# Second gate of a two-layer expert network: the transposed rows become the stationary operand, nine short products a tile

## The chip, the cores and the metric

One core of one Trainium2 chip. The metric is the device time of one launch in microseconds, median of three runs. TensorE multiplies (weight loads shown apart from the matmuls), VectorE and ScalarE move and transform tiles, GpSimd gathers and scatters rows, SyncE issues loads.

## The reference, cut to what matters

```python
logits = x @ w_gate                                    # x: 3072 x 384, w_gate: 384 x 8
noise_scale = np.log1p(np.exp(x @ w_noise))            # w_noise: 384 x 8
noisy_logits = logits + noise_scale * noise
top2 = np.argpartition(-noisy_logits, 2, axis=1)[:, :2]
...
for e in range(E):                                     # 8 experts, 1024 hidden columns
    for k in range(2):
        mask = top2[:, k] == e
        h = np.maximum(x[mask] @ w1[e], 0.0)
        out[mask] += top2_w[mask, k, None] * (h @ w2[e])
```

Ahead of it stand a recurrent attention (4 batches, 8 heads, 768 steps, head width 48) and a first expert layer in which each token goes to one expert. The `x` of the excerpt is that layer's output. All arrays are float32. Both gates must choose the same experts as the float32 reference, so the second gate is computed with split operands: each float32 value is written as a rounded float32r part (`hi`) and the rest (`lo`), and hi x hi, hi x lo and lo x hi are added.

## The kernel before, in words

The kernel has four stages in time: attention in 24 chunks of 128 tokens (to about 178 us), the first expert layer (to about 407), the second gate with its choice and tables (to about 487), and the second expert layer (to the end). There is no planner: every engine has its own hand-written program, and semaphores order the engines. A wait is written into the program of the engine that waits, and an engine works its program strictly in order.

The second gate works on G = 24 tiles of 128 rows and 384 columns (CC = 3 blocks of 128). SyncE loads them in 12 transfers of two tiles into `gx`, a ring of NGL = 3 groups of GT = 4 tiles, once the first layer's rows are all written (`s_rows`). For each tile t:

- `gate_turn(t)` (TensorE, L1585) transposes three blocks into one of three PSUM banks (`gxT_ps`, ring of NGT = 3). It waits for the vector engine's copy of tile t - 3 (`s_gcopy`).
- ScalarE copies the bank to `gx_hi` in float32r (L804), and VectorE subtracts to get `gx_lo` (L1282).
- `gate_product(t)` (TensorE, L1597) follows two tiles behind `gate_turn`. The stationary operand is `gate_split`: 16 columns of weights' high part and 16 of their low part (gate and noise weights together make 16). The moving operand is the transposed tile, 128 columns: three products with `gx_hi` against all 32 columns, three with `gx_lo` against the first 16. The result has logits in rows and tokens in columns, 512 tokens to a bank (banks 2 to 4).
- Every four tiles ScalarE copies such a bank to `logits_T` (L798), and `gate_back` (TensorE, L1607) brings it to tokens in rows: each 128 tokens of `logits_T` are stationary, and `both`, two 16 x 16 identities above one another, is moving. This adds the two halves. It is a float32 product, which TensorE runs in two passes. The result lands in bank 6, 16 columns a tile.

VectorE then reads bank 6 once (L1285, multiplied with the first layer's gate value), and a chain of small instructions on VectorE and ScalarE picks the two experts of each token, counts, and makes the tables that the gathers of the second layer need. SyncE issues the second layer's first weight loads when tile 23 has been turned (L468).

Other lines that the argument uses: L1476 to L1561 are TensorE's attention products, all plain float32; L1561 is the first gate (stationary `y_T` 128 x 128, moving 8 columns), L1499 has 128 moving columns, L1524 has stationary blocks of 64 columns and 48 moving ones, L1545 is a bf16 product with 12 moving columns, L1555 and L1570 are transposes. L1660 to L1662 are the three float32r products of the expert layers.

Of the kernel before, what the change touches and what calls it, by code (L numbers as in the profile page):

```python
# [16 lines left out]
F32 = mybir.dt.float32  # L17
F32R = mybir.dt.float32r
BF16 = mybir.dt.bfloat16
# [8 lines left out]
def attention_moe_moe(nc, HP, D, w_T, kv_T, small_T, modality_T, modality_bias, w1_1, w2_1, w1_2, w2_2, out):  # L28
# [25 lines left out]
    GB = GT * NGL  # L54
    NHOT = 3

    GATE_ORDER = [(0, 0)] + [(1, m) for m in range(CC)] + [(0, m) for m in range(1, CC)]
    assert ET <= EC <= (B - EB) * NC and ES + 3 <= SURE[0] and EB * NC == 12
    assert D < HS and C % P == 0 and NC % (2 * NIN) == 0 and G % GB == 0 and GB % NGT == 0
    CX = C + 2  # L60
# [2 lines left out]
    with ctx:  # L63
        def sb(name, shape, dt=F32):
            return ctx.enter_context(nc.sbuf_tensor(name, shape, dt))
# [41 lines left out]
        gx_lo = [sb(f"gx_lo{i}", [P, CC, P], F32R) for i in range(NGT)]  # L107
        sb("gap", [P, 16])
        gate_split = sb("gate_split", [P, CC, 4 * E], F32R)
        both = sb("both", [4 * E, 2 * E])  # L110
        logits_x = sb("logits_x", [P, G, E])
        logits = sb("logits", [P, G, E])
        tmp_e = sb("tmp_e", [P, G, E])
# [23 lines left out]
        low_i = sb("low_i", [P, 2 * G], I32)  # L137
        low = sb("low", [P, 2 * G], BF16)
        high = sb("high", [P, 2 * G], BF16)
        with nc.sbuf_tensor("logits_T", [4 * E, GB * P], F32) as logits_T, \  # L140
                nc.sbuf_tensor("x_hi", [P, CC, R], F32R) as x_hi, nc.sbuf_tensor("x_lo", [P, CC, R], F32R) as x_lo:
            pass
        low_hot = sb("low_hot", [P, 2 * G, P], BF16)
# [130 lines left out]
        s_gw, s_ghi = sem("s_gw"), sem("s_ghi")  # L274
        s_gload = [[sem(f"s_gload{i}{h}") for h in range(2)] for i in range(NGL)]
        s_gT, s_gcopy, s_gmm = sem("s_gT"), sem("s_gcopy"), sem("s_gmm")
        s_glT, s_gback = sem("s_glT"), sem("s_gback")
        s_route = sem("s_route")
        s_ask = [sem(f"s_ask{l}") for l in range(2)]
        s_answer = [sem(f"s_answer{l}") for l in range(2)]  # L280
# [437 lines left out]
        @block.scalar  # L718
        def _(act):
            prime(act, [s_ktok, s_xl, s_carry, s_ytok])  # L720
            prime(act, [s_glT], NGL)
            prime(act, s_xst, 16)
            act.dma_start(small[:, :], small_T).then_inc(s_u, 16)
            act.dma_start(bias_all[:, :, :], modality_bias.partition_broadcast(P)).then_inc(s_small, 16)
# [62 lines left out]
            for l in range(2):  # L787

                if l == 1:
                    for i in range(2):  # L790
                        act.wait_ge(s_xst[i], 16 + 16 * (G // 2))
                    act.wait_ge(s_ask[0], 1)
                    act.activation(tmp_f[:, :, :], tmp_e[:, :, :], ACT.Exp).then_inc(s_answer[0], 1)
                    def logits_copy(q):
                        act.wait_ge(s_gmm, (q + 1) * GT + NGT)
                        act.wait_ge(s_gback, q + 1)
                        n = q % NGL
                        act.activation(logits_T[:, n * GT * P:(n + 1) * GT * P], ps[0:4 * E, 2 + n, :], ACT.Copy)\  # L798
                           .then_inc(s_glT, 1)

                    for t in range(G):
                        act.wait_ge(s_gT, t + 1)
                        act.wait_ge(s_gmm, t + 1)
                        act.activation(gx_hi[t % NGT][:, :, :], gxT_ps[t % NGT], ACT.Copy).then_inc(s_ghi, 1)  # L804
                        if t >= GT and t % GT == NGT - 1:
                            logits_copy(t // GT - 1)
                    logits_copy(G // GT - 1)
                    act.wait_ge(s_ask[1], 1)
                    act.activation(tmp_f[:, :, :], raw2[:, :, E:2 * E], ACT.Exp).then_inc(s_answer[1], 1)
                    act.wait_ge(s_answer[1], 1)  # L810
                    act.activation(scale2[:, :, :], tmp_f[:, :, :], ACT.Ln, bias=1.0).then_inc(s_answer[1], 1)
                    act.wait_ge(s_ask[1], 2)
                    act.activation(exp2[:, :], denom[:, :], ACT.Exp).then_inc(s_answer[1], 1)

                def row_hot(q):
                    part = slice(q * G, (q + 1) * G)
                    act.wait_ge(s_is[l], q + 1)
                    last = act.activation(high_hot[:, part, 0, 0:NTX[l]], high_is[:, part, 0:NTX[l]], ACT.Copy,
                                          scale=row_1[:, 0:1])
                    if l == 1:  # L820
                        for g in range(q * G + G // 2, (q + 1) * G):
                            last = act.activation(high_hot[:, g, 1, 0:NTX[l]], high_is[:, g, 0:NTX[l]], ACT.Copy,
                                                  scale=float(g))
                    last.then_inc(s_hota[l], 1)


                def hidden_high(s, q):
                    act.wait_ge(s_h[l], s * 4 + q + 1)
                    act.activation(hid_hi[:, 2 * q:2 * q + 2, :], h_ps[q], ACT.Relu).then_inc(s_hhi[l], 1)  # L829

                def step_slot(j, u):
                    s = j * 2 + u
                    if not runs_from(l, s):
                        for q in range(4):
                            hidden_high(s, q)
                        if s == 0:
                            row_hot(0)
                        return
                    hidden_high(s, 0)
                    if isinstance(s, int) and s == (ES - 1, 0)[l]:  # L840
                        act.wait_ge(s_table[l], (2, 3)[l])
                    run = lookup(act, slot_run[l], s, E - 1)
                    change, fresh = lookup(act, w1_now[l], s, 1), lookup(act, w2_now[l], s, 1)
                    for q in range(4):
                        if q:
                            hidden_high(s, q)
                        with act.If(change > 0):
                            split_w1(l, run + 1, q)
                    with act.If(fresh > 0):
                        if not isinstance(s, int) or s > 0:  # L850
                            act.wait_ge(s_o[l], s * 2)
                            act.nop(nofuse=True)
                        for a in (1, 0):
                            split_w2(l, run + 1, a)

                if l == 1:
                    row_hot(0)
                    for q in range(4):
                        split_w1(1, 0, q)
                    row_hot(1)  # L860
                    for a in (1, 0):
                        split_w2(1, 0, a)
                slots(act, l, step_slot, 2)
# [3 lines left out]
        def _(dve):  # L867
# [184 lines left out]
            def gate_parts():  # L1052

                dve.wait_ge(s_const, 5)
                dve.wait_ge(s_u, 16)
                link(dve.tensor_copy(gate_split[:, :, 0:2 * E], gate_w[1][:, :, :]))
                link(dve.tensor_tensor(gate_split[:, :, 2 * E:4 * E], gate_w[1][:, :, :], gate_split[:, :, 0:2 * E],
                                       ALU.subtract))
                link(dve.tensor_tensor(both[:, :], ident[0:4 * E, 0:2 * E], ident[0:4 * E, 2 * E:4 * E], ALU.add))
                dve.sem_inc(s_gw, 1)  # L1060

            def pick_best(at, end):
# [210 lines left out]
            for l in range(2):  # L1273
                K, NSl, KG = TOPK[l], NTX[l], TOPK[l] * G

                if l == 1:
# [3 lines left out]
                    for t in range(G):  # L1280
                        dve.wait_ge(s_ghi, t + 1)
                        dve.tensor_tensor(gx_lo[t % NGT][:, :, :], gxT_ps[t % NGT], gx_hi[t % NGT][:, :, :],  # L1282
                                          ALU.subtract).then_inc(s_gcopy, 1)
                    dve.wait_ge(s_gback, NGL + G // GT)
                    link(dve.tensor_tensor(raw2[:, :, :], ps[:, 6, 0:G * 2 * E].rearrange("p (g e) -> p g e", e=2 * E),  # L1285
                                           gate1[:, :].unsqueeze(2).to_broadcast([P, G, 2 * E]), ALU.mult))
                    dve.sem_inc(s_ask[1], 1)
# [172 lines left out]
        def _(pe):  # L1460
            prime(pe, [s_y], 2)
            prime(pe, [s_gmm], NGT)
            prime(pe, [s_gback], NGL)
            pe.wait_ge(s_const, 3)

            def head_on(tile, h):
# [109 lines left out]
            for l in range(2):  # L1576
# [11 lines left out]

                def gate_product(t):

                    q = t // GT
                    if t % GT == 0:
                        pe.wait_ge(s_glT, q + 1)
                    pe.wait_ge(s_gcopy, t + NGT + 1)
                    for n, (lo, m) in enumerate(GATE_ORDER):
                        rows = 2 * E if lo else 4 * E
                        last = pe.matmul(ps[0:rows, 2 + q % NGL, (t % GT) * P:(t % GT + 1) * P],  # L1597
                                         gate_split[:, m, 0:rows], (gx_lo if lo else gx_hi)[t % NGT][:, m, :],
                                         start=(n == 0), stop=(n == 2 * CC - 1))
                    last.then_inc(s_gmm, 1)  # L1600

                def gate_back(q):

                    pe.wait_ge(s_glT, q + NGL + 1)
                    for t in range(q * GT, (q + 1) * GT):
                        at = (t - q * GT + q % NGL * GT) * P
                        last = pe.matmul(ps[:, 6, t * 2 * E:(t + 1) * 2 * E], logits_T[:, at:at + P], both[:, :],  # L1607
                                         start=True, stop=True)
                    last.then_inc(s_gback, 1)

                if l == 1:
                    pe.wait_ge(s_gw, 1)
                    for t in range(G + NGT - 1):
                        if t < G:
                            gate_turn(t)
                        if t >= NGT - 1:
                            gate_product(t - (NGT - 1))
                        if t >= GT + NGT and t % GT == NGT % GT:
                            gate_back((t - NGT) // GT - 1)
                    gate_back(G // GT - 1)  # L1620

                if l == 1:
                    pe.wait_ge(s_chosen[1], 1)
# [172 lines left out]
```

## Time and profile before

| | us |
|---|---|
| median of three runs (lowest, highest) | 985.83 (985.77, 986.16) |
| the profiled execution's own time | 985.47 |
| its span, first to last instruction | 983.7 |
| TensorE matmuls busy | 906.2 (92%) |
| VectorE busy | 540.5 (55%) |
| ScalarE busy | 230.3 (23%) |
| GpSimd busy | 349.9 (36%) |
| mean granted TensorE clock | 0.967 |

The profile is of one execution. PE is TensorE's matmuls, PEld its weight loads, which overlap with matmuls; a matmul's duration contains its latency, so the distance between starts of like instructions says more of the rate than the duration. DVE is VectorE, ACT ScalarE, SP SyncE. The granted clock is 1.00 at 2.4 GHz and 0.50 at 1.2 GHz.

### The profile page before, as it was taken

What the parts mean: (1) busy time and instruction counts of PE and PEld (TensorE: products, weight loads), DVE (VectorE), ACT (ScalarE), POOL (GpSimd) and SP (SyncE); (2) the same over time, 40 slices, a digit from 0 to 9 for tenths busy, and PEclk for the clock granted to TensorE, in tenths of its full rate; (3) what the DMA queues carried; (4) which work ended last, traced back from release to release, by engine and by line L of the source; (5) the groups of instructions that cost most, each with busy time, mean ns of one, the idle gap of its engine ahead of it and who ended that gap; (6) DMA issues with size and microseconds to landing.
All of it is one profiled execution on the core that took longest, in us unless ns stands there. A gap on an engine that the chain in (4) does not pass through costs nothing.

```text
span 983.7 us, 22470 instructions
## 1 busy us (share of the span) xinstructions
PE 906.2 (92%) x7285; PEld 876.3 (89%) x7286; DVE 540.5 (55%) x968; ACT 230.3 (23%) x435; POOL 349.9 (36%) x364
## 2 busy tenths in 40 slices
PE   5999999999999999591499999999999999999995
PEld 5888887999999999591399999999999999999995
DVE  8888999784333343257663544435435454443532
ACT  2232333112011121054221222203213131221210
POOL 7333334324221313101542433423443424334232
PEclk9999999999999999895699999999999999999998
DMA  6676782219111112253253534525334443522233
GB/s 250 193 229 228 257 289 92 65 44 390 50 50 33 56 40 57 69 178 119 50 186 73 122 103 112 110 36 127 96 56 104 115 109 108 116 33 52 47 48 50
DMA packets 54594, 111.69 MB, mean 114 GB/s; under 512 B 8704, under 2 KB 35712, under 8 KB 54528
## 3 DMA queue, kind: packets, MB, share of 16 engines
q1 hardware_dynamic: 34896, 71.27, 21.7%
q0 software_dynamic: 15744, 34.70, 17.3%
q10 hardware_dynamic: 3888, 4.89, 1.4%
q8 instruction: 35, 0.57, 0.3%
q14 instruction: 31, 0.25, 0.1%
HBM read 84.84 MB, written 26.00 MB: 113 GB/s over the span
## 4 chain that ended last, share of the span: by engine, by line
PE 82%; DVE 12%; issue 3%; DMA 1%; DVEq 1%; ACT 1%; POOL 0%; POOLq 0%
PE ps L1660 22%; PE ps L1662 21%; PE ps L1661 21%; PE ps L1570 3%; PE ps L1530 2%; PE ps L1534 2%; PE ps L1476 2%; DVE grow L898 2%; PE ps L1499 2%; PE ps L1561 1%; DVE scores L913 1%; PE ps L1585 1%; PE ps L1597 1%; PE ps L1524 1%; DVE rest L883 1%
## 5 line engine op out<-in xcount | busy, mean ns | idle before, releaser
L1660 PE MATMUL ps<-x_hi,weights 128*128 128x256 f32 x984 | 279.1, 284 | 4.6 <-DVE x_lo L1374 2.6
L1662 PE MATMUL ps<-x_hi,weights 128*128 128x256 f32 x984 | 278.5, 283 | 0.0
L1661 PE MATMUL ps<-x_lo,weights 128*128 128x256 f32 x984 | 278.2, 283 | 0.0
L829 ACT ACTIVATE hid_hi<-ps 128x512 fp32r<-128x512 f32 x164 | 98.0, 598 | 539.7 <-PE ps L1662 533.1
L1379 DVE SCALAR_TENSOR_TENSOR hid_lo<-ps,hid_hi 128x512 fp32r<-128x512 f32 x164 | 112.8, 690 | 194.2 <-ACT hid_hi L829 172.5
L1660 PE MATMUL ps<-weights,hid_hi 128*128 (+1 forms) x616 | 214.2, 348 | 1.2 <-DVE hid_lo L1379 1.2
L1662 PE MATMUL ps<-weights,hid_lo 128*128 (+1 forms) x616 | 207.3, 336 | 0.0
L1661 PE MATMUL ps<-weights,hid_hi 128*128 (+1 forms) x616 | 207.2, 336 | 0.0
L1660 PEld LDWEIGHTS ps<-x_hi,weights 128*128 128x128 f32 x984 | 187.4, 190 | 6.6 <-issue 6.5
L1661 PEld LDWEIGHTS ps<-x_lo,weights 128*128 128x128 f32 x984 | 187.4, 190 | 0.0
L1662 PEld LDWEIGHTS ps<-x_hi,weights 128*128 128x128 f32 x984 | 187.2, 190 | 0.0
L563 POOL COPY src_now<-src_row 128x2 int32 (+1 forms) x44 | 11.3, 257 | 304.3 <-DVE row_mix L1366 174.9
L1660 PEld LDWEIGHTS ps<-weights,hid_hi 128*128 128x128 f32 x616 | 115.7, 188 | 2.2 <-issue 1.6
L1661 PEld LDWEIGHTS ps<-weights,hid_hi 128*128 128x128 f32 x616 | 115.8, 188 | 0.0
L1662 PEld LDWEIGHTS ps<-weights,hid_lo 128*128 128x128 f32 x616 | 115.5, 188 | 0.0
L677 POOL DMA_INDIRECT out_dram<-sy,dst_now x56 | 89.8, 1604 | 47.2 <-DVE sy L1392 29.8
L567 POOL DMA_INDIRECT sx<-moe_rows,src_now x62 | 64.9, 1047 | 35.0 <-POOL src_now L563 24.8
L1372 DVE CAST x_hi<-ps 128x384 fp32r<-128x384 f32 x86 | 47.4, 552 | 27.2 <-PE ps L1570 27.0
L1392 DVE TENSOR_TENSOR sy<-ps,row_mix 128x384 f32<-128x384 f32 x56 | 28.6, 553 | 48.8 <-PE ps L1662 48.7
L1570 PE MATMUL ps<-ident,sx 128*128 128x128 f32 x258 | 43.2, 277 | 11.2 <-DMA sx<-moe_rows,src_now 8.8
L1374 DVE TENSOR_TENSOR x_lo<-ps,x_hi 128x384 fp32r<-128x384 f32 x86 | 48.0, 558 | 3.0
L636 POOL TENSOR_TENSOR weights<-stage,weights 128x1536 f32 (+1 forms) x9 | 31.5, 3500 | 50.1 <-ACT weights L782 50.1
(281 smaller groups left out, 1064.4 us busy)
## 6 DMA issues: line engine op xcount, KB each, us to landing
stage<-in_moe_w_dram SPq DMA_DIRECT2D x18, 1536.0 KB, 8.2
kv_in<-in_kv_T_dram SPq DMA_DIRECT2D x24, 512.0 KB, 5.7
kv_in<-in_kv_T_dram SPq DMA_DIRECT2D x24, 448.0 KB, 3.4
w_in<-in_w_T_dram SPq DMA_DIRECT2D x24, 258.5 KB, 4.2
out_dram<-zeros SPq DMA_DIRECT2D x26, 192.0 KB
x_rows<-y_tok ACTq DMA_DIRECT2D x24, 192.0 KB
stage<-moe_rows SPq DMA_DIRECT2D x12, 384.0 KB, 4.2
stage<-in_moe_w_dram SPq DMA_DIRECT2D x2, 768.0 KB, 7.7
```

Of the source, the lines that this page charges most:

```text
L567: pool.indirect_dma_start(out=sx[u][:, t, 0:width], out_offset=None, in_=rows, in_offset=bass.IndirectOffsetOnAxis(ap=src_now[u][:, t:t + ...
L636: pool.tensor_tensor(weights[:, bass.ds(to + W2_LO, HALF)], w2_raw[:, HALF:WSZ], weights[:, bass.ds(to + W2_HI, HALF)], ALU.subtract).then ...
L677: pool.indirect_dma_start(out=out, out_offset=where, in_=sy[u][:, t, 0:C], in_offset=None, compute_op=ALU.add).then_inc(s_scatter[l][u][t] ...
L829: act.activation(hid_hi[:, 2 * q:2 * q + 2, :], h_ps[q], ACT.Relu).then_inc(s_hhi[l], 1)
L1372: dve.tensor_copy(x_hi[:, :, part], x_T).then_inc(s_xhi[l], 1)
L1374: dve.tensor_tensor(x_lo[:, :, part], x_T, x_hi[:, :, part], ALU.subtract).then_inc(s_sxc[l], 1)
L1379: dve.scalar_tensor_tensor(hid_lo[:, part, :], h_ps[q], 0.0, hid_hi[:, part, :], ALU.max, ALU.subtract).then_inc(s_hlo[l], 1)
L1392: dve.tensor_tensor(sy[u][:, t, 0:C], o_ps[t], row_mix[:, bass.ds(s * TS + t, 1)].to_broadcast([P, C]), ALU.mult).then_inc(s_oc[l], 1)
L1570: last = pe.transpose(x_T[:, c, :], sx[u][:, t, c * P:(c + 1) * P], ident[:, :])
L1660: pe.matmul(out_ps, hi, by_hi, start=first, stop=False)
L1661: pe.matmul(out_ps, hi, by_lo, start=False, stop=False)
L1662: return pe.matmul(out_ps, lo, by_hi, start=False, stop=final)
```

## The change

`gate_product` swaps its operands. The transposed tile (`gx_hi` or `gx_lo`, one block of 128 x 128) is stationary, and 16 columns of `gate_split` move. For each of the three blocks there are three products: hi with the weights' high part, hi with their low part, lo with their high part; nine accumulate in bank 6, tokens in rows. `gate_back`, `logits_copy`, `logits_T`, `both` and the semaphores `s_glT` and `s_gback` go. VectorE's read of bank 6 now waits for the last `gate_product`. The tensor `first_half` only keeps the place in memory that `logits_T` had; the tensors behind `both` move by 64 bytes a partition.

```diff
-    GATE_ORDER = [(0, 0)] + [(1, m) for m in range(CC)] + [(0, m) for m in range(1, CC)]
+    GATE_ORDER = [(x, w, m) for m in range(CC) for x, w in ((0, 0), (0, 1), (1, 0))]
...
-        both = sb("both", [4 * E, 2 * E])
...
-        with nc.sbuf_tensor("logits_T", [4 * E, GB * P], F32) as logits_T, \
+        with nc.sbuf_tensor("first_half", [P, G, P], BF16), \
...
-                    def logits_copy(q):
-                        act.wait_ge(s_gmm, (q + 1) * GT + NGT)
-                        act.wait_ge(s_gback, q + 1)
-                        n = q % NGL
-                        act.activation(logits_T[:, n * GT * P:(n + 1) * GT * P], ps[0:4 * E, 2 + n, :], ACT.Copy)\
-                           .then_inc(s_glT, 1)
...
-                        if t >= GT and t % GT == NGT - 1:
-                            logits_copy(t // GT - 1)
-                    logits_copy(G // GT - 1)
...
-                link(dve.tensor_tensor(both[:, :], ident[0:4 * E, 0:2 * E], ident[0:4 * E, 2 * E:4 * E], ALU.add))
...
-                    dve.wait_ge(s_gback, NGL + G // GT)
+                    dve.wait_ge(s_gmm, NGT + G)
...
-                    q = t // GT
-                    if t % GT == 0:
-                        pe.wait_ge(s_glT, q + 1)
                     pe.wait_ge(s_gcopy, t + NGT + 1)
-                    for n, (lo, m) in enumerate(GATE_ORDER):
-                        rows = 2 * E if lo else 4 * E
-                        last = pe.matmul(ps[0:rows, 2 + q % NGL, (t % GT) * P:(t % GT + 1) * P],
-                                         gate_split[:, m, 0:rows], (gx_lo if lo else gx_hi)[t % NGT][:, m, :],
-                                         start=(n == 0), stop=(n == 2 * CC - 1))
+                    for n, (x, w, m) in enumerate(GATE_ORDER):
+                        last = pe.matmul(ps[:, 6, t * 2 * E:(t + 1) * 2 * E], (gx_hi, gx_lo)[x][t % NGT][:, m, :],
+                                         gate_split[:, m, w * 2 * E:(w + 1) * 2 * E],
+                                         start=(n == 0), stop=(n == 3 * CC - 1))
                     last.then_inc(s_gmm, 1)
...
-                def gate_back(q):
-
-                    pe.wait_ge(s_glT, q + NGL + 1)
-                    for t in range(q * GT, (q + 1) * GT):
-                        at = (t - q * GT + q % NGL * GT) * P
-                        last = pe.matmul(ps[:, 6, t * 2 * E:(t + 1) * 2 * E], logits_T[:, at:at + P], both[:, :],
-                                         start=True, stop=True)
-                    last.then_inc(s_gback, 1)
...
-                        if t >= GT + NGT and t % GT == NGT % GT:
-                            gate_back((t - NGT) // GT - 1)
-                    gate_back(G // GT - 1)
```

## Rows read from the trace of the kernel before

**Rows 1.** The page: TensorE's busy tenths in 40 slices of 24.6 us.

```profile
PE   5999999999999999591499999999999999999995
```

**Rows 2.** The chain that ended last, 417 to 446 us: start, us, what.

```profile
418.10 2.24 PE ps L1585 x9
...
426.14 0.36 PE ps L1597 x6
426.50 0.33 PE ps L1585 x3
...
428.61 1.01 PE ps L1607 x8
...
430.11 0.36 PE ps L1597 x6
...
441.52 0.84 PE ps L1597 x12
...
443.03 1.07 PE ps L1607 x8
...
444.13 0.57 DVE raw L1285
```

**Rows 3.** Instructions in order of time, 424 to 441 us, VectorE and SyncE.

```profile
426.70 1.94 DVE L1282 TENSOR_TENSOR gx_lo<-ps,gx_hi 128x384 fp32r<-128x384 f32 x3 [1.19 <-ACT gx_hi L804]
...
440.18 0.38 SPq L413 DMA_DIRECT2D stage<-in_moe_w_dram  x1
```

**Rows 4.** Weight loads by line and shape: count, busy us, mean ns, idle before.

```profile
L1660 PEld LDWEIGHTS ps<-x_hi,weights 128*128 128x128 f32 x984 | 187.4, 190 | 6.6 <-issue 6.5
...
L1561 PEld LDWEIGHTS ps<-small,y_T 128*128 128x128 f32 x192 | 23.3, 192 | 2.2 <-issue 2.2
...
L1555 PEld LDWEIGHTS ps<-ident,y_T 128*128 128x128 f32 x96 | 10.9, 142 | 2.9 <-DVE y_T L967 2.4
...
L1597 PEld LDWEIGHTS ps<-gx_hi,gate_split 128*32 128x32 f32 x72 | 6.7, 110 | 0.9 <-issue 0.3
...
L1545 PEld LDWEIGHTS ps<-early_hot,low_hot 128*128 128x128 bf16 x12 | 0.4, 96 | 0.0
```

**Rows 5.** TensorE in order of time, attention stage, 60 to 68 and near 160.

```profile
65.62 0.97 PEld L1561 LDWEIGHTS ps<-small,y_T 128*128 128x128 f32 x8
...
66.54 1.14 PE L1499 MATMUL ps<-rk,u_block 128*128 128x128 f32 x8
...
160.15 0.45 PE L1545 MATMUL ps<-early_hot,low_hot 128*128 128x12 bf16 x12
```

**Rows 6.** Stretches in the gate: us, PE busy (count), granted clock, DMA share, GB/s.

```profile
418.10:420.90 2.80, 2.80 (x15) 0.50 1.04 373
420.90:421.20 0.30, 0.30 (x5) 0.71 1.08 405
421.20:424.60 3.40, 3.40 (x45) 1.00 1.01 323
```

**Rows 7.** The same columns for stretches of attention and first experts.

```profile
138.00:140.00 2.00, 1.13 (x11) 1.00 1.08 401
...
162.00:164.00 2.00, 0.92 (x9) 1.00 0.00 0
...
165.10:168.40 3.30, 3.30 (x27) 0.50 0.16 55
...
176.00:178.00 2.00, 1.45 (x12) 1.00 0.45 139
...
178.80:182.10 3.30, 3.30 (x18) 0.50 0.49 136
```

**Rows 8.** Weight loads in order of time, half clock, then full.

```profile
11.71 1.83 PEld L1499 LDWEIGHTS ps<-rk,u_block 128*128 128x128 f32 x8
13.77 0.94 PEld L1524 LDWEIGHTS ps<-kv_in,k_tok 128*64 128x64 f32 x16 [0.23 <-issue]
...
61.00 0.55 PEld L1524 LDWEIGHTS ps<-kv_in,k_tok 128*64 128x64 f32 x16 [0.28 <-issue]
```

More of the change, by code:

```diff
@@ L276, in attention_moe_moe @@
         s_gT, s_gcopy, s_gmm = sem("s_gT"), sem("s_gcopy"), sem("s_gmm")
-        s_glT, s_gback = sem("s_glT"), sem("s_gback")
         s_route = sem("s_route")
@@ L720, in _ @@
             prime(act, [s_ktok, s_xl, s_carry, s_ytok])
-            prime(act, [s_glT], NGL)
             prime(act, s_xst, 16)
@@ L1462, in _ @@
             prime(pe, [s_gmm], NGT)
-            prime(pe, [s_gback], NGL)
             pe.wait_ge(s_const, 3)
```

## The prediction

> **What bounds the kernel now.** I read the page's slices first: TensorE is at 9 tenths nearly throughout, but slices 17 to 20 read 5, 9, 1, 4 [rows 1]. Those slices lie between the two expert layers, where the second gate works. Whatever its length, everything behind it (noise, choice of two experts, tables, first gathers) starts when its logits are in PSUM, and no expert product can run before that. So the change is worth what it does to the interval from the first turned tile (418.10) to the vector engine's read of the logits (444.13), one for one.
>
> The chain of waits through that interval [rows 2] is TensorE's own work and nothing else. The reader is to see a pattern: 0.33 us for three transposes (L1585), 0.36 for the six products of a tile (L1597), and after every fourth tile 1.01 us for eight passes that turn the logits back (L1607), behind which the next transposes start slowly: four tiles take 430.11 - 426.14 = 3.97 us, 4 x 0.69 + 1.2. At the end, 12 products (0.84), a gap to 443.03 in which ScalarE makes its last copy, and eight more passes (1.07). The vector engine's subtraction (L1282) keeps pace; three of them last 1.94, so one starts each (1.94 - 0.56) / 2 = 0.69 us [rows 3]. It is paced by the tiles; its own work is 0.56.
>
> **What is taken away.** Six groups of turning passes at 1.2 us beside the transposes, of which the last is 1.07 alone, and the last copy with its hand-over (441.52 + 0.84 = 442.36 to 443.03, 0.67): 5 x 1.2 + 0.67 + 1.07 = 7.7 us. Also the six products of each tile, 0.36. The five other ScalarE copies lie beside TensorE work and give nothing. The vector instruction that made `both` (32 x 16 elements) stood in the first expert layer, where TensorE is at 9 tenths with its own products [rows 1] and VectorE's small work lies beside them: nothing; without that cover it would be some 0.2 us. No DMA is moved. The weight load that SP issues behind the last transpose (440.18, [rows 3]) stood 3.95 us ahead of the read of the logits; now three tiles' products lie between, at least as long at either clock, so it starts no later against all that follows.
>
> **What is added.** Nine products a tile with 128 x 128 stationary data and 16 moving columns. The trace has no such float32r product, so its spacing is bounded from neighbours. The stationary load is what must be paid each time. Float32r loads of 128 columns last 190 ns in the expert loop and the plain float32 loads of L1561 192; the gate's own loads of 32 columns last 110 [rows 4]. So float32r loads like float32, by columns. L1561 is the near twin, a full stationary tile with 8 moving columns: 8 loads in 0.97, (0.97 - 0.19) / 7 = 0.111 us each [rows 5]. L1607 gives the same (8 in 1.01 to 1.07, a matmul's latency in it, [rows 2]). Upper bound at this clock: the same loads with 128 moving columns, L1499, (1.14 - 0.28) / 7 = 0.124 [rows 5]. Lower bound: the bf16 products of L1545, 12 in 0.45, (0.45 - 0.17) / 11 = 0.026 [rows 5]; their loads last 96 ns, not 190 [rows 4]. I take 0.11, by the twin. A tile is then 3 + 9 = 12 x 0.11 = 1.32 us where it was 0.69. (If a transpose's load, 142 against 192 ns [rows 4], lets it start earlier, 1.26; with 0.124, 1.45.)
>
> The Trainium skill, page "TensorE: Matmul & The Clock Gate", section on LDWEIGHTS, gives the load as columns over 1.2 GHz, 107 ns for 128; with that figure a tile would be about 1.3 us by estimate, and the twin's 0.111 agrees. The same page, on fast weight load, says that loads of 128 weights that are not FP32 go faster; the 190 ns row speaks against counting float32r among them, and by that rule the sum would fall below today's (rival 2).
>
> *Sum at 2.4 GHz.* Turned tiles 0 to 2 unchanged, to 420.34. The clock is half until about 421.1 (0.50 up to 420.9, 0.71 in the next 0.3 us, [rows 6]), so tile 0's nine cost about 1.4 us. Then 21 tiles x 1.32 = 27.7, the last two 18 x 0.11 = 2.0, a matmul's latency 0.2: 420.34 + 31.3 = 451.6, which is 7.5 us later than 444.13.
>
> **The clock.** This is where I had to choose. The granted clock rises near 421.1 after nine transposes and the first 128-column products, and stays 1.00 while TensorE streams 128 columns in every instruction of a tile [rows 6]. In the changed kernel only 3 of 12 instructions of a tile stream 128 columns; 9 stream 16, and the array waits for loads. What does such a stretch do? The trace has none longer than 0.9 us, but two places come near. At 162 to 165, after a pause (0.92 busy of 2.00), the eight short products of L1561 lead, and the clock is at 0.50 from 165.1, though 128-column passes had begun behind them. At 176.0 to 178.8 TensorE runs four transposes, the eight short products, a pause and the first expert products: 0.50 again [rows 7]. Both times the clock came back behind solid 128- and 256-column passes (3.30 busy of 3.30). Against that, the stretch from 138, with a longer pause (1.13 busy of 2.00) and the same short products, but with eight 128-column passes whole behind them, kept 1.00 [rows 7]. I read these as: what lifts and holds the clock is streaming, and a load with 16 columns behind it is poor in that. Each near place has idle time, so this is a reading and no proof; the other reading (busy is enough) is rival 1.
>
> At 1.2 GHz, loads of 128 columns start 0.213 us apart: L1499 near 12 us, 8 loads in 1.83, (1.83 - 0.34) / 7. Those also stream 128 columns; a row where the load alone counts is L1524, whose pairs of 64-column loads come (0.94 - 0.22) / 7 = 0.103 apart at half clock against (0.55 - 0.14) / 7 = 0.059 at full [rows 8], so 128 columns are about 0.206. I take 0.213. Transposes are 0.213 to 0.249 (nine in 2.24, [rows 2]). Tile: 12 x 0.213 = 2.56 us, between 2.45 and 2.66.
>
> *Sum at 1.2 GHz.* In the kernel before, tile 0's six 128-column products and the next transposes came just ahead of the rise; now short ones stand there, so I expect no rise at all in the gate. 420.34 + 9 x 0.213 (1.9) + 21 x 2.56 (53.8) + 18 x 0.213 (3.8) + 0.35 latency = 480.2. That is 36.1 us later. Behind it TensorE pauses in either kernel, and the later stages keep their rows. VectorE (0.56 a tile, [rows 3]) and the ScalarE copy ahead of it lie beside 2.56. Loads of the rows have more time than they need.
>
> The profiled execution took 985.47 us (span 983.7, 1.8 around it), 0.36 under the median 985.83. 985.47 + 36.1 = 1021.6; against the median 1021.9. I forecast **1022 us**, 3.7% slower. Own range: tile 2.45 to 2.66 gives 21 x 0.1 = 2.2 us either way, with the start and the rise another 2: 1018 to 1026.
>
> **Rivals.**
> 1. *The clock rises at 421 and stays.* For: TensorE has practically no idle time in the new gate, and the falls seen all had pauses. Against: the near places above. Time: +7.5 us, 993.3, with tiles of 1.26 to 1.45 giving 992 to 996. The Trainium skill, same page, section on why this matters for your kernels, says that an engine kept continuously busy goes to full speed and pauses take it back; by that rule this rival holds, with 993 us. The rows above do not decide it: no stretch there is both free of pauses and full of short products.
> 2. *Float32r loads of 128 columns go fast.* One mechanism, the other sign. From 420.34 to 444.13 there are 23.8 us; 21 x 3 x 0.11 = 6.9 are transposes, leaving 16.7 for about 216 product slots: below 0.077 us each the change wins. At the bf16 row's 0.026 a tile's TensorE work would be 0.56, and VectorE's pace of at most 0.69 would bind: 420.34 + 0.6 + 21 x 0.69 + 0.6 = 436, 8 us faster, 978; at 0.06 about 3 us faster, 982.5. Against: 190 ns in [rows 4], the same as float32.
> 3. *The clock goes up and down within the gate,* for stretches with transposes bunched. Half and half: about +22, 1008.
>
> **Chances.** Forecast 0.60, rival 1 0.28, rival 3 0.06, rival 2 0.04; 0.02 for spacing that happens to meet today's time. To leave out at most 2 in 10 the range has to reach rival 1: 991.5 to 1026. What a measurement here can tell from no change is about 0.2%, 2 us. Faster 0.04, same 0.02, slower 0.94: every case but rival 2 adds more than 7 us.
>
> **What would show it.** In the profile after: the loads of L1597's successor, 216 of them (9 x 24) with 128 columns, 0.33 us long at half clock or 0.19 at full; the granted clock from 421 to the end of the gate, 0.50 (forecast) or 1.00 (rival 1); the interval from the first transpose to the read of the logits, 62 us, 33.5 us, or under 26 (rival 2); no wait on ScalarE or VectorE inside it. Everything ahead of 418 and behind the read keeps its length within 1 us. The prediction is wrong if the clock holds, if the loads are not 0.11 or 0.21 apart, or if the stage behind the gate changes length because loads of the second layer's weights now come at another time.

## The result, and the profile after

| | before | after |
|---|---|---|
| median, us (lowest, highest; runs) | 986.0 (985.77, 989.17; 4) | 1021.63 (1020.89, 1022.34; 4) |
| ratio, with its 95% interval | | 1.033 (1.031 to 1.036) |
| the profiled execution's own time | 985.47 | 1022.22 |
| its span | 983.7 | 1020.5 |

The changed kernel is 3.3% slower; its 1021.63 us lie 0.4 under the forecast of 1022. I read its profile in the order of the one before. First the page: TensorE's busy line and, under it, the granted clock, in 40 slices.

```profile
PE   6999999999999999598259999999999999999995
...
PEclk9999998999999999655569999999999999999998
```

A slice is now 25.5 us. In [rows 1] slices 17 to 20 read 5, 9, 1, 4; now slices 17 to 21 read 5, 9, 8, 2, 5: TensorE works for some one slice and a half longer between the two expert layers (944.1 us busy against 906.2, both from the page), and the clock line shows fives there. The chain of waits says with what (start, us, what):

```profile
409.79 0.57 DVE sy L1376
...
417.16 4.70 DMA stage<-moe_rows
...
421.90 0.90 PE ps L1570 x3
422.81 1.72 PE ps L1578 x9
424.52 0.75 PE ps L1570 x3
425.28 1.72 PE ps L1578 x9
...
473.99 0.75 PE ps L1570 x3
474.75 5.57 PE ps L1578 x27
480.34 0.57 DVE raw L1271
```

L1570 is `gate_turn`, L1578 the new `gate_product`, L1271 the vector engine's read of the logits. The pattern of [rows 2], 0.33 and 0.36, has become 0.75 and 1.72, one tile each 2.47 us, twenty-one times without a gap and without an entry of ScalarE or VectorE between. The chain puts the border between two groups where one ends; the starts of the instructions give the terms more plainly (TensorE in order of time, a transpose group, the first products behind it, the next transposes):

```profile
441.69 0.90 PE L1570 MATMUL ps<-ident,stage 128*128 128x128 f32 x3
442.24 0.57 PE L1578 MATMUL ps<-gate_split,gx_hi 128*128 128x16 f32 x2
...
444.16 0.90 PE L1570 MATMUL ps<-ident,stage 128*128 128x128 f32 x3
```

From the first of the nine products to the next transposes it is 1.92 us, 0.213 a product, and the three transposes take 0.55. The view of the tile `gate_split` gives the loads and products one by one (duration lowest/median/highest in ns, first and last start, shape):

```profile
L1578 PEld LDWEIGHTS ps<-gate_split,gx_hi x144: 333/333/337, 422.4 to 479.7; 128*128 128x128 f32 x144
...
L1578 PEld LDWEIGHTS ps<-gate_split,gx_lo x72: 333/333/333, 422.8 to 479.9; 128*128 128x128 f32 x72
```

All 216 loads last 333 ns, from the first to the last; none shows the 190 ns that such a load has at 2.4 GHz [rows 4]. The granted clock in two stretches of the gate (us, busy and count of PE, PEld, DVE, ACT, POOL, granted clock, DMA share, GB/s):

```profile
424.60:430.00 5.40, 5.40 (x28) 5.40 (x27) 1.11 (x2) 0.98 (x2) 0.00 (x0) 0.50 0.60 186
440.00:450.00 10.00, 10.00 (x51) 10.00 (x50) 2.23 (x4) 1.96 (x4) 0.00 (x0) 0.50 0.25 79
```

TensorE is busy for every microsecond of them, as is its weight load, and the clock is 1.2 GHz. Busy is meant as the profile counts it: a product here lasts 0.361 us in the trace and the next one starts after 0.213, so the row is full although, as the experiments below show, each product waits for a load.

**The sum against the profile.** Cut at the first `gate_product` (420.34 before, from [rows 2], 422.81 after) and at the read of the logits (444.13 and 480.34): ahead of the cut +2.47 us; between, 57.53 against 23.79, +33.74; behind, 541.88 against 541.34 to the end of the execution, +0.54. Together 36.75, which is 1022.22 - 985.47. The forecast had 0, 59.9 - 23.8 = +36.1, and 0. So the gate was 2.3 us shorter than forecast and the rest 3.0 us longer, under a total that is right to 0.7 us.

The 2.47 us came before the gate. The last instruction of the first layer's sums starts at 409.79; in the trace of before it started at 407.05. TensorE is already 2.7 us later at the first expert product (181.08 against 178.34), so the time was lost in the attention. Three rows of TensorE's windows of after, for stretches of the attention (us, PE busy and count, clock, DMA share, GB/s):

```profile
138.00:140.00 2.00, 1.28 (x12) 1.00 1.10 405
140.50:143.80 3.30, 3.30 (x27) 0.50 0.95 307
...
164.40:170.90 6.50, 6.50 (x42) 0.50 0.09 33
```

and the second stretch in the kernel before:

```profile
140.50:143.80 3.30, 3.30 (x44) 1.00 0.92 304
```

In [rows 7] the stretch from 138 kept its clock in the kernel before; here the clock is lost behind it, and 27 instructions fit where 44 did. The fall near 165 of [rows 7] lasts 6.5 us in place of 3.3. At the first gate's products behind the pause of 162 the kernel after is 1.1 us late (164.20 against 163.08), and 2.7 at the first expert product. The instructions of that stage are the same in both; only the place of some tensors differs, by 64 bytes a partition. The traces of the experiments below, whose code there is that of the kernel after, put the last instruction of the sums at 406.39 to 411.59, and in one of them, six_wide, the clock did not fall between 136 and 186 us (all engines):

```profile
136.00:186.00 50.00, 43.40 (x481) 38.35 (x480) 44.94 (x65) 17.06 (x39) 24.42 (x22) 1.00 0.42 139
```

The repeated runs of the kernel before alone went from 985.2 to 992.5 us. The variation between runs is enough to explain the 2.7 us; nothing here shows a part of the change in it.

### The profile page after: what moved, and what is told of

Read it like the earlier page. It is cut to its first block, busy times and chain, and to the rows that moved or that the text cites. A ratio compares the mean times of both kernels' runs of the same rounds, so it can differ in the third digit from the quotient of the medians.

```text
span 1020.5 us, 22497 instructions
## 1 busy us (share of the span) xinstructions
PE 944.1 (93%) x7309; PEld 915.2 (90%) x7310; DVE 540.3 (53%) x967; ACT 227.8 (22%) x429; POOL 347.9 (34%) x364
## 4 chain that ended last, share of the span: by engine, by line
PE 84%; DVE 9%; issue 2%; DMA 1%; DVEq 1%; ACT 0%; POOL 0%; POOLq 0%; SPq 0%
PE ps L1629 21%; PE ps L1631 21%; PE ps L1630 21%; PE ps L1578 4%; PE ps L1555 3%; PE ps L1515 2%; PE ps L1519 2%; PE ps L1484 2%; PE ps L1461 2%; PE ps L1570 2%; PE ps L1546 2%; PE ps L1509 1%; DVE grow L885 1%; PE ps L1469 1%; PE ps L1540 1%
```

## The experiments

Three theories are tried: **load** (nine stationary loads are the tile's length, at whatever clock is granted), **streaming** (the clock stays at 1.2 GHz because 16 columns behind a load are poor in streaming; my forecast), **busy** (a TensorE without pauses keeps or gets 2.4 GHz; rival 1). All but the one named otherwise start from the kernel after. The kernel before, timed beside them on the same chip, took 988.51 us with lift, lift_hold, wide and bf16_rows, 987.62 with wide256, six_loads, six_wide and back_twice, and 988.47 with bf16_again; it was 986.0 with the kernel after. The ratios are against these, and a difference of two times from different groups is uncertain by some 2 us.

**1. lift.** Fifty bf16 products of 512 columns ahead of the gate, so that it begins at 2.4 GHz.

```diff
                 if l == 1:
+                    for n in range(50):
+                        pe.matmul(ps[:, 2, :].rearrange("p (a b) -> p a b", a=4), ones_b[:, :],
+                                  causal_b[:, :].unsqueeze(1).to_broadcast([P, 4, P]), start=True, stop=True)
                     pe.wait_ge(s_gw, 1)
```

> The changed kernel with 50 bf16 products of 512 moving columns into an unused bank, run while TensorE waits for the gate's first rows, so that the gate begins at the full clock. Theory (nine loads with 16 columns behind each neither lift nor hold the clock): the granted clock is 1.00 at the gate's start and falls to 0.50 inside it, most of the 24 tiles still take 2.4 to 2.5 us; 1017 to 1021 us. Rival (busy is enough to hold it, only the rise was missed): 1.00 through the gate, tiles of 1.25 to 1.32 us, about 991 us.

One run: 1028.11 us. The windows, all engines:

```profile
432.40:435.90 3.50, 3.44 (x32) 3.44 (x32) 1.50 (x4) 1.10 (x3) 0.00 (x0) 1.00 0.19 22
436.10:440.00 3.90, 3.90 (x21) 3.90 (x20) 0.92 (x2) 0.87 (x2) 0.00 (x0) 0.50 0.44 165
440.00:487.00 47.00, 47.00 (x229) 47.00 (x228) 10.03 (x18) 8.44 (x18) 0.00 (x0) 0.50 0.21 62
```

and the chain of waits:

```profile
411.56 6.04 issue
417.60 13.29 PE ps L1585 x50
430.89 0.34 PE ps L1570 x3
431.26 0.50 ACT gx_hi L794
...
431.85 0.57 DVE gx_lo L1268
...
433.63 0.40 PE ps L1570 x3
434.04 0.91 PE ps L1578 x9
...
436.35 0.75 PE ps L1570 x3
437.11 1.72 PE ps L1578 x9
```

The first row is TensorE before the fillers (here L1585), the next the fillers themselves, and then tiles at either clock. At 2.4 GHz a tile is 0.40 + 0.91 = 1.31 us, the 1.32 of the forecast's sum for that clock; at 1.2 GHz it is 2.47 again. By the starts, the tile at 2.4 GHz is 0.30 us of transposes and 1.01 of nine products, 0.112 each:

```profile
433.49 0.54 PE L1570 MATMUL ps<-ident,stage 128*128 128x128 f32 x3
433.79 0.37 PE L1578 MATMUL ps<-gate_split,gx_hi 128*128 128x16 f32 x2
...
434.80 0.55 PE L1570 MATMUL ps<-ident,stage 128*128 128x128 f32 x3
```

The clock fell at about 436 though TensorE had been busy for 3.44 of the 3.50 us ahead, and did not come back in 47 us of unbroken work. The fall alone would leave a doubt, since the fillers and the first products are parted by a pause of half a microsecond in which ScalarE and VectorE make the first operands (431.26 to 432.42 in the chain, with transposes in part of it). The 47 us behind it leave none. That refutes the busy theory: work without pauses was not enough to give the clock back. The time missed its expectation for another reason: the fillers started 6 us after the last expert product and took 13.29 us, so the gate's first product began at 432.46, 9.7 us later than in the kernel after (422.81).

**2. lift_hold.** The same, and one more such 512-column product behind each tile's nine.

```diff
                             gate_product(t - (NGT - 1))
+                            pe.matmul(ps[:, 2, :].rearrange("p (a b) -> p a b", a=4), ones_b[:, :],
+                                      causal_b[:, :].unsqueeze(1).to_broadcast([P, 4, P]), start=True, stop=True)
```

> As lift, and one bf16 product of 512 columns (0.22 us at full clock) behind every tile's nine. Theory: the added streaming holds the clock at 1.00, a tile takes 1.25 to 1.32 plus 0.22 to 0.25, some 1.5 us, and the kernel is faster than the changed one although it does more: 996 to 1000 us. If the short products pull the clock down whatever stands beside them: tiles of 2.9 us, 1031 us. If busy is enough (rival), also about 998, but then lift is at 991.

1031.98 us, ratio 1.044 (1.041 to 1.047). A miss for streaming as I had sized it; the other case of the expectation (the clock falls all the same, tiles of 2.9 us, 1031) came. The windows:

```profile
428.60:432.10 3.50, 3.46 (x31) 3.31 (x31) 1.48 (x3) 0.78 (x3) 0.00 (x0) 1.00 0.16 9
...
436.00:491.00 55.00, 55.00 (x255) 51.30 (x254) 10.04 (x18) 8.84 (x18) 0.00 (x0) 0.50 0.18 56
```

The clock fell at 432.1, no later in the gate than in lift. The long product of a tile did not hold it; it adds 0.47 us a tile less what the transposes give back (0.64 + 1.72 + 0.47 = 2.83).

**3. wide.** The same nine loads, each with 128 moving columns: the 16 weights' columns, eight times over, by a broadcast. Each tile overwrites the places of the next ones.

```diff
-                        last = pe.matmul(ps[:, 6, t * 2 * E:(t + 1) * 2 * E], (gx_hi, gx_lo)[x][t % NGT][:, m, :],
-                                         gate_split[:, m, w * 2 * E:(w + 1) * 2 * E],
+                        last = pe.matmul(ps[:, 6, t * 2 * E:(t + 8) * 2 * E].rearrange("p (a e) -> p a e", a=8),
+                                         (gx_hi, gx_lo)[x][t % NGT][:, m, :],
+                                         gate_split[:, m, w * 2 * E:(w + 1) * 2 * E].unsqueeze(1).to_broadcast([P, 8, 2 * E]),
```

> The changed kernel with the same nine products and the same stationary loads, each moving the 16 weight columns eight times over (128 columns; the result of a tile is right in its first 16 columns, the others are overwritten by the next tile). Theory: the clock rises near the third tile and stays at 1.00; loads come 0.11 to 0.125 us apart, tiles of 1.3 to 1.45 us, 992 to 997 us: eight times the columns and 25 to 30 us faster. Rival (the loads of float32r rows are slow by themselves at 0.21 us, or the clock needs something else): no gain, 1021 us or more.

1021.32 us, ratio 1.032 (1.030 to 1.035). Again a miss for streaming as I had sized it, and a hit for load:

```profile
424.00:440.00 16.00, 16.00 (x80) 16.00 (x79) 3.35 (x6) 3.27 (x7) 0.00 (x0) 0.50 0.37 117
440.00:479.00 39.00, 39.00 (x190) 39.00 (x190) 8.36 (x15) 7.06 (x15) 0.00 (x0) 0.50 0.15 49
```

Eight times the columns change neither the clock nor the tile (0.66 + 1.81 = 2.47): they fit behind the load.

**4. bf16_rows, and 9. bf16_again.** The split rows and weights in bf16 instead of float32r. The products' count and shapes stay; the logits are coarser, and some of the choices may differ.

```diff
-        gx_hi = [sb(f"gx_hi{i}", [P, CC, P], F32R) for i in range(NGT)]
-        gx_lo = [sb(f"gx_lo{i}", [P, CC, P], F32R) for i in range(NGT)]
+        gx_hi = [sb(f"gx_hi{i}", [P, 2 * CC, P], BF16)[:, 0:CC, :] for i in range(NGT)]
+        gx_lo = [sb(f"gx_lo{i}", [P, 2 * CC, P], BF16)[:, 0:CC, :] for i in range(NGT)]
...
-        gate_split = sb("gate_split", [P, CC, 4 * E], F32R)
+        gate_split = sb("gate_split", [P, CC, 8 * E], BF16)
```

> The changed kernel with the split parts of the rows and of the gate weights in bf16 in place of float32r (this changes the precision of the gate's logits and so some choices of experts; 216 products as before). Theory (the stationary load is the term): loads of 96 ns, some 0.03 us apart at full clock, and TensorE no longer sets the pace: tiles of about 0.69 us set by the copies, gate some 9 us shorter than before the change, 975 to 981 us. If it is the number of products that costs: tiles of 1.3 or 2.5 us, 993 or 1021.

> The same kernel as bf16_rows (split parts of rows and gate weights in bf16, a coarser gate), timed in more rounds against the kernel before the change. The load as the term gives 8 to 10 us less than before the change on any chip: 977 to 981 us where the kernel before takes 986 to 988. If the first timing was luck with the clock in the stages ahead of the gate, a ratio within 0.3% of 1.

979.73 us, ratio 0.991 (0.988 to 0.994), and in the second run of the same kernel 980.28, ratio 0.992 (0.989 to 0.994). The tile's view, the chain and the windows of the first of the two:

```profile
L1578 PEld LDWEIGHTS ps<-gate_split,gx_hi x144: 94/96/152, 420.2 to 437.9; 128*128 128x128 bf16 x144
```

```profile
423.18 0.23 PE ps L1578 x9
423.41 0.73 PE ps L1570 x3
...
428.80 0.22 PE ps L1578 x9
429.02 0.38 PE ps L1570 x3
```

```profile
423.00:426.50 3.50, 3.50 (x48) 3.31 (x47) 1.67 (x3) 1.87 (x4) 0.00 (x0) 0.50 0.67 240
426.60:438.00 11.40, 10.83 (x209) 8.95 (x208) 9.48 (x17) 7.84 (x16) 0.00 (x0) 1.00 0.52 144
```

The first pair of chain rows is at 1.2 GHz, the second at 2.4. Nine products cost 0.23 us where the float32r ones cost 1.72 at the same clock and with the same columns: with wide, where eight times the columns cost nothing, this shows that the stationary operand's load is what the change pays for. Freed of it, the new form of the gate is faster than the old one, at the times that rival 2 gave (978 to 982.5). From the end of the first layer to the read of the logits the two took 30.4 and 28.9 us (407.74 to 438.16, 408.46 to 437.40) against 37.1 in the kernel before (407.05 to 444.13), so the gain lies in this stretch. The clock rose in it as well, with the same columns a tile as in the kernel after. The old form of the gate was not run in bf16, so how much of the gain is the swap and how much the type is not shown.

**5. wide256.** As wide, with 256 columns, into two banks, so that VectorE reads the logits in two instructions.

```diff
...
-                        last = pe.matmul(ps[:, 6, t * 2 * E:(t + 1) * 2 * E], (gx_hi, gx_lo)[x][t % NGT][:, m, :],
-                                         gate_split[:, m, w * 2 * E:(w + 1) * 2 * E],
+                        q, at = t // (G // 2), t % (G // 2) * 2 * E
+                        last = pe.matmul(ps[:, (2, 6)[q], at:at + 256].rearrange("p (a e) -> p a e", a=16),
+                                         (gx_hi, gx_lo)[x][t % NGT][:, m, :],
+                                         gate_split[:, m, w * 2 * E:(w + 1) * 2 * E].unsqueeze(1).to_broadcast([P, 16, 2 * E]),
```

> As wide, but each of the nine products moves the 16 weight columns sixteen times over (256 columns; tiles 0 to 11 land in one bank, 12 to 23 in another, and the vector engine reads the two in two instructions). Theory, mended after wide and lift_hold (it is still streaming that lifts the clock, only 128 columns in every 0.21 us are too few at half clock): 256 columns fill the time between loads, the clock rises after some three or four tiles and stays; tiles 2.5 us before, 1.4 us after; 997 to 1003 us. Rival (streaming does not matter, the swapped operands hold the clock down in another way): 0.50 throughout, 1021 to 1023 us.

998.25 us, ratio 1.010 (1.006 to 1.015): some 23 us faster than the kernel after (ratio 1.033), with sixteen times its moving columns. Windows and chain:

```profile
422.90:426.20 3.30, 3.30 (x17) 3.30 (x17) 0.81 (x2) 0.49 (x1) 0.00 (x0) 0.50 0.72 242
426.30:457.00 30.70, 30.70 (x260) 30.70 (x260) 11.15 (x20) 9.84 (x20) 0.00 (x0) 1.00 0.28 90
```

```profile
424.93 1.72 PE ps L1582 x9
426.65 0.33 PE ps L1573 x3
426.98 1.10 PE ps L1582 x9
```

Here the clock rises at 426.3 and stays to the end of the gate, and a tile is 1.43 us. Nothing but the columns (and the second bank and read that they need) differs from wide, which stayed at 0.50: what streams does bear on the clock.

**6. six_loads and 7. six_wide.** One load of `gx_hi` serves both halves of the weights (32 columns), so a tile has six loads; the low half is added by two more vector instructions behind the gate. six_wide repeats those columns eight times (`rpt` = 8; 256 and 128 columns).

```diff
...
-                    for n, (x, w, m) in enumerate(GATE_ORDER):
-                        last = pe.matmul(ps[:, 6, t * 2 * E:(t + 1) * 2 * E], (gx_hi, gx_lo)[x][t % NGT][:, m, :],
...
+                    rpt, at = 1, t % 8 * 4 * E
+                    out_t = ps[:, 2 + t // 8, at:at + rpt * 4 * E].rearrange("p (a e) -> p a e", a=rpt)
+                    for m in range(CC):
+                        pe.matmul(out_t, gx_hi[t % NGT][:, m, :],
+                                  gate_split[:, m, :].unsqueeze(1).to_broadcast([P, rpt, 4 * E]),
...
+                        last = pe.matmul(out_t[:, :, 0:2 * E], gx_lo[t % NGT][:, m, :],
+                                         gate_split[:, m, 0:2 * E].unsqueeze(1).to_broadcast([P, rpt, 2 * E]),
...
```

> The changed kernel with six products a tile in place of nine: hi of the rows against both halves of the weights in one product (32 moving columns), lo against the first half (16); the two halves are added by the vector engine (two more instructions of some 0.6 us). Theory (the stationary load is the price, the clock stays at 0.50): each load less saves 0.21 us, a tile takes 1.83 us, 1006 to 1009 us. If something other than the number of loads sets the tile: less than 5 us gained.

> As six_loads, with the columns moved eight times over (256 with hi, 128 with lo). Theory: the clock rises after about three tiles of 1.83 us and stays, tiles of 1.05 to 1.1 us after that; 988 to 993 us, within 0.6% of the kernel before the change. Rival (no rise): 1006 to 1009 us as six_loads.

six_loads took 1007.32 us, ratio 1.020 (1.015 to 1.024), and six_wide 991.15 us, ratio 1.003 (1.001 to 1.005). The window of six_loads:

```profile
424.00:464.00 40.00, 40.00 (x198) 40.00 (x197) 11.69 (x21) 10.29 (x21) 0.00 (x0) 0.50 0.25 78
```

and those of six_wide:

```profile
418.70:421.70 3.00, 2.99 (x15) 2.99 (x16) 1.42 (x3) 0.98 (x3) 0.00 (x0) 0.50 0.99 356
421.80:443.00 21.20, 21.20 (x193) 21.20 (x193) 11.69 (x21) 10.00 (x21) 0.00 (x0) 1.00 0.39 118
```

Three loads fewer take a tile from 2.47 to 1.83 us at the same clock, 0.213 each, which is the spacing that the forecast took from the attention [rows 8]. The two kernels have the same loads and differ in columns alone; with the wide ones the clock is 1.00 from 421.8 on, and the stretch from the end of the first layer to the read of the logits takes 37.22 us where the kernel before takes 37.08.

**8. back_twice.** The kernel before, each group of turning passes run twice, to price what the change takes away.

```diff
-                    for t in range(q * GT, (q + 1) * GT):
+                    for t in [t for _ in range(2) for t in range(q * GT, (q + 1) * GT)]:
```

> The kernel before the change with each group of turning passes run twice (16 passes in place of 8, six times). Prices the removed work alone: 8 passes at 0.11 to 0.13 us, 0.9 to 1.0 us six times, 5.4 to 6.2 us more than the kernel before. If they were hidden behind the copies: no change.

994.89 us, ratio 1.007 (1.004 to 1.010), which is 4 to 10 us more than the kernel before. The chain has five groups of 1.91 or 1.92 us, one of 1.97:

```profile
424.52 1.92 PE ps L1607 x16
...
447.39 1.97 PE ps L1607 x16
```

Each is 0.9 us longer than in [rows 2]. From the end of the first layer to the read it took 42.70 us, 5.6 more than before. The eight passes of a group therefore cost 0.9, all six groups 5.6 of the 7.7 us that the forecast took off. The rest, the slow transposes behind each group and the last copy, is read from [rows 2] and had no experiment of its own.

## Why the prediction was right, step by step

**What bounds the gate: right.** From the first transpose to the read of the logits it took 60.35 us, where I had given 62. That was the whole difference but for what varies between runs, and no wait on ScalarE or VectorE entered the chain.

**What is taken away, 7.7 us: right as far as it was tried**, 5.6 of it by back_twice.

**The spacing of loads, 0.11 us at 2.4 GHz and 0.213 at 1.2: right.** By the starts it was 0.112 in lift, and 0.213 in the kernel after and between six and nine loads. That it is the load and not the product was an inference from twins. wide shows it, where only the product became longer, and bf16_rows agrees, where the type and with it the load changed (96 ns in place of 333 or 190). The row of 190 ns [rows 4] was the right evidence against rival 2.

**The tile, 12 x 0.213 = 2.56: a little high.** 2.47 was measured. The nine products took the 1.92 us of the sum, but the three transposes 0.55 in place of 0.64. That is near the lower bound that I gave (2.45). The shorter load of a transpose, which I had named as a possible saving at the full clock, fits: here it lasts 0.224 us against 0.333 (medians in the kernel after). Over the gate it is 2.3 us: 57.5 measured against 59.9.

**The clock, 0.50 throughout: right, and the reason half right.** Lift shows that a busy TensorE is not enough; the pair six_loads and six_wide, and wide256, show that the same loads get another clock with more columns behind them. How much streaming that takes I had wrong: by my expectations 128 columns to a load, or one product of 512 in a tile, should have held the clock, and neither did. bf16_rows got the full clock with the columns of the kernel after, once its loads were short, so the columns of a tile are not the whole of it either. The two near places of the attention [rows 7] pointed the right way, but had pauses in them, which the gate has not, and the contrast that I drew with the stretch from 138 does not stand: with the same instructions behind a pause of the same length (1.13 us before, 1.14 after), the kernel before kept its clock there and the kernel after lost it. The Trainium skill, page "TensorE: Matmul & The Clock Gate", section "Why this matters for your kernels", would keep the clock by continuous activity; the traces disagree for this kind of work, with 47.00 busy of 47.00 us at 0.50 in lift.

**Everything ahead of 418 within 1 us: wrong.** The first transpose moved by 1.9 us (419.99), the end of the first layer by 2.7, since the clock was low in the attention for longer: once more near 140, and for 6.5 us in place of 3.3 near 165. I had put this term at nothing, and the traces of one and the same attention code differ in it by 5 us (406.39 to 411.59), so one profiled run of it can't be held to 1 us. It was luck that this made up for the tile.

**Everything behind the read within 1 us: right,** 0.54 us longer.

What stays open: why the clock falls in the attention in some runs and not in others, and what exactly the clock follows; the runs only show the cases named.

## What to carry to other kernels

- A product with a full float32r stationary operand costs its load, here 0.11 us at 2.4 GHz or 0.21 at 1.2, however few columns move. Swapping operands to save a transposition of the result multiplies these loads; count loads, not multiplications. Here 6 small loads a tile became 9 large ones to save 7.7 us, and even at the full clock that would have lost (1.31 us a tile in lift against 0.69).
- A stage that waits for loads can also lose the clock, and then its float32r terms nearly double (1.31 to 2.47 us a tile). Look at the granted clock of the nearest such stretch before summing; columns repeated to no other use can be the cheaper way (wide256, 23 us).
- Where the precision allows bf16, the swap and the type together pay (0.991), since nine loads and products then take 0.23 us; bf16 without the swap was not tried.

## What was unexpected of the hardware

- Moving 128 columns in place of 16 in each of 216 products cost nothing measurable (1021.32 against 1021.63 us), clock and load spacing being the same.
- Nine bf16 products took 0.23 us at 1.2 GHz and 0.21 to 0.22 at 2.4 in two tiles of three (0.37 in the third; TensorE stood idle for `gx_lo` ten times there, 2.7 us in all): unlike the float32r ones, they hardly followed the clock in this chain.
- The same attention code lost the full clock at different places from trace to trace, and in six_wide nowhere between 136 and 186 us.
- In lift, TensorE stood 6.04 us between its last expert product and the first filler, which waits for no other engine; the profile calls it issue. Its cause was not looked into.
